# Which side of a runtime branch stands first: the same two blocks in the other order on three engines

## The chip, the cores and the metric

The kernel runs on one core of a Trainium2 chip. Its measure is the device time of one launch in microseconds (us). Each engine of the core (TensorE, VectorE, ScalarE, GpSimd, SyncE) has its own instruction stream and runs it in order; between engines only semaphores order the work. Instructions are fetched from memory while the program runs, and the profile shows these fetches as DMA queues of their own kind, "instruction".

## The reference

Three stages in float32: attention, a soft mixture of 8 experts, and a gated layer.

```python
scores = scale * q @ k.T                         # 2 x 8 heads, 768 positions, 64 wide
keep = (pos_k < n_sink) | ((rel >= 0) & (rel < window))
a = softmax(where(keep, scores, -1e9));  x = a @ v
P = exp(x @ w_gate - max);  8 times: rows, then columns normalised
out = sum over e of P[:, e] * (relu(x @ w1[e]) @ w2[e])
return ((out @ w_a) * (out @ w_b)) @ w_out
```

`n_sink` and `window` are inputs, here 4 and 128. With at most 16 sinks and a window of 1 to 129 the non-zero part of the scores is a narrow band and 16 columns; with other values it can be anything.

## The kernel before, in words

Since the two sizes are known only on the device, the kernel holds two forms of the attention stage. VectorE reads the sizes, computes `in_range` (1 when the band form is valid), and raises `range_ready`. Each engine then calls `chosen`, which waits for it and loads the value into a register. Two tests follow on each engine: `If(fits == 0)` with the general block (one head at a time over all 768 keys, in loops) and then `If(fits == 1)` with the sink-and-band block. For the inputs timed here the first test fails and the second holds. An engine therefore jumps over its general block, and runs through the sink-and-band block behind it into the rest.

The sink-and-band block handles 8 pairs of heads. Queries and keys are split into a high and a low part (ScalarE L956 and L958 make the high one, VectorE L1258 and L1261 the low one), TensorE multiplies three parts per tile of 128 queries (L541), VectorE adds the mask and takes the row minimum (L1272), ScalarE applies the exponential (L967), GpSimd and VectorE normalise, TensorE transposes (L567) and multiplies with the values (L588, L595). Ahead of the first pair VectorE also makes the mask: L1234 and L1236, then L1242 and L1245. Pairs overlap: while pair p is transposed, the scores of p + 2 are made.

Behind the branch TensorE makes the router's logits (L648), which VectorE copies out (L1373); then come the experts, in groups of 14 products (L623 to L625) on weight parts that VectorE and ScalarE split (L1336, L948) and whose results VectorE adds (L1535). Experts 1 to 6 run in a hardware loop of six turns (L1652 on VectorE, L824 on TensorE). SyncE issues the loads; those of the next weights wait for the splits of the last (`w_lo`). One wait inside the last step of the block matters below: L1331 is held until L1325 has ended (`t_sum`).

On VectorE the general block takes 280 rows of the program order (rows of equal neighbours are merged), on TensorE 117, on ScalarE 25, on SyncE 24, on GpSimd 8.

Of the kernel before, what the change touches and what calls it, by code (L numbers as in the profile page):

```python
# [33 lines left out]
def build(nc, qT, kT, v, sizes, w_gate, w1, w2, w_a, w_b, w_out, out):  # L34
    B, H, D, S = qT.shape
# [5 lines left out]
    KC = DM // P  # L41
# [14 lines left out]
    LEAD = 2  # L56
    RING = 4
    PAIRS = HEADS // 2
# [19 lines left out]
    with ctx:  # L78
        def sem(name):
            return ctx.enter_context(nc.semaphore(name))  # L80
# [92 lines left out]
        s = {n: sem(n) for n in names}  # L173
# [114 lines left out]
        @block.sync  # L288
        def _(sp):
            def load_pair(i, b):  # L290

                row = batch_rows(i, b)
                if i > 0:
                    sp.wait_ge(s["qk_lo"], 2 * (B * i + b - 1))
                sp.dma_start(rk[:, b].rearrange("d (t n) -> d t n", n=PITCH)[:, :, 0:P],
                             kT_rows[bass.ds(row, P), :].rearrange("d (t n) -> d t n", n=P))\
                    .then_inc(s[f"qk_in{b}"], 16)
                sp.dma_start(rq[:, b, :], qT_rows[bass.ds(row, P), :]).then_inc(s[f"qk_in{b}"], 16)

            def load_values(b):  # L300

                sp.dma_start(vs[:, b], v_rows[b][:, :, 0:P]).then_inc(s[f"v_in{b}"], 16)
                sp.wait_ge(s["sink_zero"], 1)
                sp.dma_start(vz[0:SINK, b], v_rows[b][0:SINK, 0, 0:P]).then_inc(s[f"v_in{b}"], 16)

            def load_w1(e, hf, sub):
                f0 = hf * FM * P + sub * SUBF
                sp.dma_start(raw1[:, sub], w1_rows[:, bass.ds(e * KC, KC), f0:f0 + SUBF])\
                    .then_inc(s[f"raw1_in{sub}"], 16)

            def load_w2(e, hf):
                sp.dma_start(raw2[:], w2_rows[:, bass.ds(e * HALVES * FM + hf * FM, FM), :])\
                    .then_inc(s["raw2_in"], 16)

            def load_step(e, hf):
                n = HALVES * e + hf
                for sub in range(2):
                    sp.wait_ge(s["w_lo"], 6 * (n - 1) + 3 * sub + 3)
                    if not isinstance(e, int):
                        sp.sem_inc(s["past"])  # L320
                    load_w1(e, hf, sub)
                sp.wait_ge(s["w2_lo"], FM * n)
                if not isinstance(e, int):
                    sp.sem_inc(s["past"])
                load_w2(e, hf)

            def general_loads(j, c, b):
                group = (j * KC + c) * B + b
                row = batch_rows(c, b)
                sp.wait_ge(s["d_lo"], 2 * group + 2)  # L330
                sp.sem_inc(s["past"])
                sp.dma_start(d_q, qT_rows[bass.ds(row, P), bass.ds(j * P, P)]).then_inc(s["d_in"], 16)
                sp.dma_start(d_k, kT_rows[bass.ds(row, P), :]).then_inc(s["d_in"], 16)
                sp.dma_start(d_v, v_rows[b][:, :, bass.ds(c * P, P)]).then_inc(s["d_in"], 16)


            sp.dma_start(ints[:], sizes.bitcast(I32).rearrange("(a n) -> a n", a=1).to_broadcast([P, 4]))\
                .then_inc(s["flags_in"], 16)
            load_pair(0, 0)
            load_pair(0, 1)  # L340
            load_values(0)
            sp.dma_start(wg[:], w_gate.rearrange("(c p) e -> p c e", p=P)).then_inc(s["gate_in"], 16)
            fits = chosen(sp)
            with sp.If(fits == 0):
                for landed in ("qk_in0", "qk_in1"):
                    sp.wait_ge(s[landed], 32)
                sp.wait_ge(s["v_in0"], 32)
                for sub in range(2):
                    load_w1(0, 0, sub)
                with sp.Fori(0, QT) as j:  # L350
                    with sp.Fori(0, KC) as c:
                        for b in range(B):
                            general_loads(j, c, b)
                sp.wait_ge(s["d_lo"], 2 * GROUPS + 2)
                load_w2(0, 0)

            with sp.If(fits == 1):
                load_values(1)
                for sub in range(2):
                    load_w1(0, 0, sub)  # L360
                for i in range(1, KC):
                    for b in range(B):
                        load_pair(i, b)
                sp.wait_ge(s["qk_lo"], 2 * PAIRS)
                load_w2(0, 0)
            load_step(0, 1)
            with sp.Fori(1, E) as e:
                load_step(e, 0)
                load_step(e, 1)

            for t in range(STEPS2):
                for sub, rows in ((0, wa_rows), (1, wb_rows)):
                    sp.wait_ge(s["w_lo"], 6 * (STEPS + t - 1) + 3 * sub + 3)
                    sp.dma_start(raw1[:, sub], rows[:, :, t * SUBF:(t + 1) * SUBF])\
                        .then_inc(s[f"raw1_in{sub}"], 16)
                sp.wait_ge(s["w2_lo"], FM * STEPS + 2 * t)
                half = 2 * (t % 2)
                sp.dma_start(raw2[:, half:half + 2], wo_rows[:, 2 * t:2 * t + 2, :]).then_inc(s["raw2_in"], 16)


            for x in range(TILES):
                t = x if x < HTILES else HTILES + ORDER[x - HTILES]
                sp.wait_ge(s["out_acc"], HTILES * (KT - B) + x + 1)
                sp.dma_start(out_rows[:, t, :], acc[:, t, :]).then_inc(s["out_sent"], 16)
            sp.wait_ge(s["out_sent"], 16 * TILES)
# [537 lines left out]
        def _(act):  # L923
# [7 lines left out]
            def gate_parts_hi():  # L931
                act.wait_ge(s["gate_in"], 16)
                nc.scalar.copy(wgs[:, :, 0:E], wg[:]).then_inc(s["gate_hi"], 1)
                nc.scalar.copy(wgs[:, :, GL:GL + E], wg[:]).then_inc(s["gate_hi"], 1)
# [15 lines left out]
            def split_pair_hi(p):  # L950
                i, b = divmod(p, B)
                q_hi, _, k_hi, _ = pair_parts(b)
                if p >= 2:
                    act.wait_ge(s["scores"], 2 * QT * (p - 1))
                act.wait_ge(s[f"qk_in{b}"], 32 * (i + 1))
                nc.scalar.copy(q_hi, rq[:, b, :]).then_inc(s["qk_hi"], 1)  # L956
                act.wait_ge(s["sinks_in"], p + 1)
                nc.scalar.copy(k_hi, rk[:, b, 0:KW]).then_inc(s["qk_hi"], 1)  # L958
# [66 lines left out]
                                     accum_out=esum[:, 0, 0:1]).then_inc(s["d_exped"], 1)  # L1025

            fits = chosen(act)
            with act.If(fits == 0):
                with act.Fori(0, QT) as j:
                    with act.Fori(0, KC) as c:  # L1030
                        for b in range(B):
                            for a in range(2):
                                general_head(j, c, b, a)
                act.wait_ge(s["d_t"], 1)
                nc.scalar.copy(xoh_op[:, 4, :], x32_op[:, 5, :]).then_inc(s["d_thi"], 1)
                act.wait_ge(s["d_t"], 5)
                nc.scalar.copy(xoh_op[:, 0:2, :], x32_op[:, 0:2, :])
                nc.scalar.copy(xoh_op[:, 3, :], x32_op[:, 3, :])
                nc.scalar.copy(xoh_op[:, 2, 0:BEFORE_LAST], x32_op[:, 2, 0:BEFORE_LAST])
                nc.scalar.copy(xoh_op[:, 5:7, 0:BEFORE_LAST], x32_op[:, 5:7, 0:BEFORE_LAST])\  # L1040
                    .then_inc(s["d_thi"], 1)
                act.sem_inc(s["t_hi"], 10)
                gate_parts_hi()
                ws_hi(0, 0, (0, 1, 2))

            with act.If(fits == 1):
                for p in range(LEAD):
                    split_pair_hi(p)
                for p in range(-LEAD, PAIRS):
                    if p == -1:  # L1050
                        gate_parts_hi()
                    pair(p)

            def gate_exp():

# [143 lines left out]
        def _(dve):  # L1199
# [223 lines left out]
                nc.vector.tensor_copy(x32_flat[rows, bass.ds(at, P)], ps[rows, O_BANK, 0:P]).then_inc(s["d_lo"], 1)  # L1423

            fits = chosen(dve)
            with dve.If(fits == 0):
                dve.wait_ge(s["d_pos"], 2)
                for jh in range(2):
                    with dve.Fori(0, QT // 2) as j3:
# [30 lines left out]
                dve.sem_inc(s["x_ready"], 1)  # L1460
                gate_parts_lo()
                ws_lo(0, 0, (0, 1, 2))

            with dve.If(fits == 1):
                in_window()
                split_pair_lo(0)
                make_mask()
                mask_scores(0, (0, 1))
                split_pair_lo(1)
                for p in range(-LEAD, PAIRS):  # L1470
                    if p == -1:
                        gate_parts_lo()
                    pair(p)


            links = 0
# [323 lines left out]
```

## Time and profile before

| | us |
|---|---|
| median of 3 runs | 1452.02 (1451.71 to 1453.65) |
| the profiled execution | 1450.18 |
| its span, first to last instruction | 1448.4 |
| TensorE busy | 1398.6 (97%) |
| VectorE busy | 808.4 (56%) |
| ScalarE busy | 501.5 (35%) |
| GpSimd busy | 223.7 (15%) |

Instruction queues in the whole span: q8 with 36 packets of 0.59 MB together, q14 with 24 of 0.20 MB. A load of half a step's weights is 512.0 KB and lands 3.4 us after its issue (median of 32).

A profile records one execution. The busy shares say which engine is full over the whole span; which engine sets the time of a short stretch is read from the chain of waits in that stretch. An idle time put down to "issue" is one for which the profile shows no semaphore that came late.

### The profile page before, as it was taken

The page shows a single profiled execution, that of the slowest core. Times are in us where ns is not written, and L with a number is a line of the kernel's source. Part 1 is how long each engine was busy: PE and PEld are TensorE (multiplying, and loading weights), DVE is VectorE, ACT ScalarE, POOL GpSimd, SP SyncE. Part 2 cuts the span into 40 slices and gives each one's busy share as a digit, 9 for nine tenths or more (in the row PEclk, how much of TensorE's full clock was granted, in tenths as well). Part 3 has the DMA queues.
Part 4 walks back from the last instruction along what each step waited for, and adds up shares of the span by engine and source line. Part 5 has one row for each costly group of instructions (what it writes and reads, how often), then busy time and mean ns, then how long its engine had stood idle before and what let it go on. Part 6 is the DMA issues. An engine that isn't in the chain of part 4 may idle for free.

```text
span 1448.4 us, 20715 instructions
## 1 busy us (share of the span) xinstructions
PE 1398.6 (97%) x7400; PEld 1246.1 (86%) x7400; DVE 808.4 (56%) x1585; ACT 501.5 (35%) x1085; POOL 223.7 (15%) x289
## 2 busy tenths in 40 slices
PE   4877999999999999999999999999999999999999
PEld 3655889988889998889998888998888989999998
DVE  6898765645444453544545444454544666656665
ACT  5785232423223242222323222242322443232331
POOL 3355110101101010110101011010111321101100
PEclk9999999999999999999999999999999999999999
DMA  4311100001010000101001010000100001001002
GB/s 141 100 45 56 44 30 29 30 29 59 15 44 29 29 29 29 58 21 37 29 29 32 26 58 29 29 29 29 58 15 29 15 30 44 30 30 44 30 1 88
DMA packets 49724, 56.45 MB, mean 39 GB/s; under 512 B 2432, under 2 KB 37376, under 8 KB 49664
## 3 DMA queue, kind: packets, MB, share of 16 engines
q1 hardware_dynamic: 44768, 53.26, 11.3%
q10 hardware_dynamic: 4896, 2.41, 0.6%
q8 instruction: 36, 0.59, 0.2%
q14 instruction: 24, 0.20, 0.0%
HBM read 52.51 MB, written 3.15 MB: 38 GB/s over the span
## 4 chain that ended last, share of the span: by engine, by line
PE 86%; DVE 7%; ACT 4%; issue 2%; DMA 0%; DVEq 0%; ACTq 0%
PE ps L623 28%; PE ps L625 28%; PE ps L624 28%; ACT pr L967 2%; DVE pr L1298 1%; DVE st L1675 1%; DVE pr L1272 1%; DVE wsl L1336 1%; PE ps L693 1%; DVE pt L1307 1%; ACT pt L976 1%; PE ps L567 0%; ACT st L1139 0%; ACT hh L1146 0%; DVE acc L1714 0%
## 5 line engine op out<-in xcount | busy, mean ns | idle before, releaser
L623 PE MATMUL ps<-xoh,wsh 128*128 128x384 f32 x1232 | 414.9, 337 | 3.0 <-DVE xol L1579 2.1
L625 PE MATMUL ps<-xol,wsh 128*128 128x384 f32 x1232 | 412.7, 335 | 0.0
L624 PE MATMUL ps<-xoh,wsl 128*128 128x384 f32 x1232 | 412.3, 335 | 0.0
L623 PE MATMUL ps<-w2h,hh 128*128 128x512 f32 x912 | 360.7, 396 | 0.8 <-DVE acc L1557 0.8
L625 PE MATMUL ps<-w2l,hh 128*128 128x512 f32 x912 | 359.8, 395 | 0.0
L624 PE MATMUL ps<-w2h,hl 128*128 128x512 f32 x912 | 359.6, 394 | 0.0
L1562 DVE SCALAR_TENSOR_TENSOR acc<-ps,g_now,acc 128x512 f32<-128x512 f32 x180 | 135.1, 751 | 201.7 <-PE ps L625 201.7
L623 PEld LDWEIGHTS ps<-xoh,wsh 128*128 128x128 f32 x1232 | 231.3, 188 | 10.5 <-DVE st L1675 3.9
L624 PEld LDWEIGHTS ps<-xoh,wsl 128*128 128x128 f32 x1232 | 231.3, 188 | 3.7
L625 PEld LDWEIGHTS ps<-xol,wsh 128*128 128x128 f32 x1232 | 231.2, 188 | 0.0
L625 PEld LDWEIGHTS ps<-w2l,hh 128*128 128x128 f32 x912 | 171.7, 188 | 39.8
L623 PEld LDWEIGHTS ps<-w2h,hh 128*128 128x128 f32 x912 | 171.9, 188 | 37.0 <-DVE acc L1557 1.2
L624 PEld LDWEIGHTS ps<-w2h,hl 128*128 128x128 f32 x912 | 171.8, 188 | 35.7
L436 POOL TENSOR_TENSOR sst<-raw 128x256 f32<-128x256 f32 x44 | 32.5, 738 | 1037.6 <-DVE wsl L1336 1037.6
L1071 ACT COPY st<-ps 128x384 f32<-128x384 f32 x96 | 46.0, 480 | 373.7 <-PE ps L625 373.7
L1535 DVE TENSOR_TENSOR st<-ps,st 128x384 f32<-128x384 f32 x96 | 53.4, 557 | 122.2 <-PE ps L625 122.2
L1535 DVE TENSOR_TENSOR ab<-ps,ab 128x384 f32<-128x384 f32 x96 | 53.5, 558 | 85.0 <-PE ps L625 84.9
L1543 DVE SCALAR_TENSOR_TENSOR hl<-ps,hh 128x384 fp32r<-128x384 f32 x64 | 35.7, 557 | 77.2 <-ACT hh L1084 76.7
L1336 DVE TENSOR_TENSOR wsl<-raw,wsh 128x512 fp32r<-128x512 f32 x88 | 63.8, 739 | 17.4 <-ACT wsh L948 17.4
L948 ACT CAST wsh<-raw 128x512 fp32r<-128x512 f32 x88 | 52.0, 621 | 55.2 <-POOL raw L438 55.2
L1084 ACT ACTIVATE hh<-ps 128x384 fp32r<-128x384 f32 x64 | 31.5, 491 | 106.1 <-PE ps L625 106.1
L1071 ACT COPY ab<-ps 128x384 f32<-128x384 f32 x96 | 46.1, 480 | 55.6 <-PE ps L625 55.6
(142 smaller groups left out, 1337.8 us busy)
## 6 DMA issues: line engine op xcount, KB each, us to landing
raw<-in_w_dram SPq DMA_DIRECT2D x32, 512.0 KB, 3.4
raw<-in_w_dram SPq DMA_DIRECT2D x16, 1024.0 KB, 5.1
rk<-in_k_dram SPq DMA_DIRECT2D x8, 384.0 KB, 4.0
rq<-in_q_dram SPq DMA_DIRECT2D x8, 384.0 KB, 4.9
raw<-in_w_a_dram SPq DMA_DIRECT2D x6, 512.0 KB, 3.6
raw<-in_w_b_dram SPq DMA_DIRECT2D x6, 512.0 KB, 3.6
raw<-in_w_out_dram SPq DMA_DIRECT2D x6, 512.0 KB, 3.5
out_dram<-acc SPq DMA_DIRECT2D x12, 256.0 KB, 2.0
```

What stands on the lines that cost most here:

```text
L436: nc.gpsimd.tensor_tensor(s1, a21, a22, ALU.add).then_inc(s["s_sum"], 1)
L623: nc.tensor.matmul(o, ah, bh, start=first, stop=False, skip_group_check=True)
L624: nc.tensor.matmul(o, al, bh, start=False, stop=False, skip_group_check=True)
L625: return nc.tensor.matmul(o, ah, bl, start=False, stop=last, skip_group_check=True)
L948: nc.scalar.copy(ws_piece(wsh, sub, j), ws_raw(sub, j)).then_inc(s["w_hi"], 1)
L967: nc.scalar.activation(t, t, ACT.Exp, bias=nmin[:, r, j:j + 1], scale=-1.0, accum_out=esum[:, r, j:j + 1]).then_inc(s["exped"], 1)
L1071: nc.scalar.copy((st, ab)[sub][:, slot, :], ps[:, bank_of(sub, name), 0:HT]).then_inc(s["kept"], 1)
L1084: nc.scalar.activation(hh[:, 2 * sub + 1, 0, :], ps[:, bank_of(sub, "P4"), 0:HT], ACT.Relu)\
L1336: nc.vector.tensor_tensor(ws_piece(wsl, sub, j), ws_raw(sub, j), ws_piece(wsh, sub, j).bitcast(F32), ALU.subtract)\
L1535: nc.vector.tensor_tensor(t, ps[:, bank_of(sub, name), 0:HT], t, ALU.add).then_inc(s["c_add"], 1)
L1543: nc.vector.scalar_tensor_tensor(out=hl[:, 2 * sub + m, half, :], in0=src, scalar=0.0, in1=hh[:, 2 * sub + m, half, :].bitcast(F32), op0=A ...
L1562: ins = nc.vector.scalar_tensor_tensor(out=acc[:, tile, :], in0=ps[:, Y_BANK + k % 2, :], scalar=g_now[:, tile:tile + 1], in1=acc[:, tile, ...
```

## The change

On VectorE, ScalarE and SyncE the two `If`s become one `If(fits == 1)` with an `Else`: the sink-and-band block stands first and the general block behind it. Nothing inside the blocks changes. TensorE and GpSimd keep the two `If`s with the general block first. In the diff the moved blocks are cut.

```diff
@@ SyncE
-            with sp.If(fits == 0):
+            with sp.If(fits == 1):
+                load_values(1)
...
+                load_w2(0, 0)
+            with sp.Else():
                 for landed in ("qk_in0", "qk_in1"):
...
-            with sp.If(fits == 1):
-                load_values(1)
...
@@ ScalarE
-            with act.If(fits == 0):
+            with act.If(fits == 1):
+                for p in range(LEAD):
+                    split_pair_hi(p)
+                for p in range(-LEAD, PAIRS):
+                    if p == -1:
+                        gate_parts_hi()
+                    pair(p)
+            with act.Else():
                 with act.Fori(0, QT) as j:
...
@@ VectorE
-            with dve.If(fits == 0):
+            with dve.If(fits == 1):
+                in_window()
+                split_pair_lo(0)
+                make_mask()
+                mask_scores(0, (0, 1))
+                split_pair_lo(1)
+                for p in range(-LEAD, PAIRS):
+                    if p == -1:
+                        gate_parts_lo()
+                    pair(p)
+            with dve.Else():
                 dve.wait_ge(s["d_pos"], 2)
...
-            with dve.If(fits == 1):
-                in_window()
...
```

The line numbers behind the blocks fall by 2 or 3 (VectorE's L1234 becomes L1232, its L1373 becomes L1371).

The order on VectorE at its first test, before: the test L1426 stands in front of the general block, and the second test L1464 in front of the band block.

```order
L202 ISA x2
L1426 COMPARE_AND_BRANCH
L1429 UNCONDITIONAL_BRANCH
L1429 ISA
...
L1336 TENSOR_TENSOR wsl<-sst,wsh 128x768
L1426 UNCONDITIONAL_BRANCH
L1464 COMPARE_AND_BRANCH
L1234 TENSOR_SCALAR pt<-pt,lim 128x672
L1236 SCALAR_TENSOR_TENSOR pt<-pt 128x672
```

The same place after the change.

```order
L202 ISA x2
L1424 COMPARE_AND_BRANCH
L1232 TENSOR_SCALAR pt<-pt,lim 128x672
L1234 SCALAR_TENSOR_TENSOR pt<-pt 128x672
L1256 TENSOR_TENSOR wsl<-rq,wsh 128x768
```

The 280 rows between the first test and the mask's first step are gone from there, and one test with them.

The order on VectorE at the end of the band block, before: the last outputs of the attention (L1331), then the copies of the logits (L1373); the unconditional branch goes to the row behind it.

```order
L1329 TENSOR_TENSOR x<-ps,x 128x384
L1331 TENSOR_TENSOR x<-ps,x 128x384
L1464 UNCONDITIONAL_BRANCH
L1373 COPY lt<-ps 40x384 x2
L1336 TENSOR_TENSOR wsl<-raw,wsh 128x512 x2
```

After: the same branch now has 279 rows between it and its target.

```order
L1327 TENSOR_TENSOR x<-ps,x 128x384
L1329 TENSOR_TENSOR x<-ps,x 128x384
L1424 UNCONDITIONAL_BRANCH
L1437 UNCONDITIONAL_BRANCH
...
L1334 TENSOR_TENSOR wsl<-sst,wsh 128x768
L1434 UNCONDITIONAL_BRANCH
L1371 COPY lt<-ps 40x384 x2
L1334 TENSOR_TENSOR wsl<-raw,wsh 128x512 x2
```

The general block has moved here from in front of the band block. On TensorE both orders are the same but for the line numbers.

## Rows read from the trace of the kernel before

**Rows 1.** The page, part 4: the chain that ended last, by engine.

```profile
PE 86%; DVE 7%; ACT 4%; issue 2%; DMA 0%; DVEq 0%; ACTq 0%
```

**Rows 2.** The waits from 0 to 24 us: who waited, total, times, longest.

```profile
PE ps L541 <- DVE wsl L1261: 14.6, 1, 14.6
DVE pt L1234 <- issue: 6.4, 1, 6.4
```

**Rows 3.** The chain from 0 to 24 us: start, duration, what.

```profile
5.90 5.29 issue
11.29 0.58 DVE pt L1234
...
13.62 0.95 DVE wsl L1261
...
15.98 0.29 DVE pr L1272
```

**Rows 4.** Branches by line: duration in ns min/median/max, first and last start in us.

```profile
L1426 DVEq COMPARE_BRANCH  x1: 67/67/67, 5.8 to 5.8; - x1
...
L1464 DVEq COMPARE_BRANCH  x1: 50/50/50, 11.2 to 11.2; - x1
...
L697 PEldq COMPARE_BRANCH  x1: 5560/5560/5560, 5.9 to 5.9; - x1
...
L1046 ACTq COMPARE_BRANCH  x1: 40/40/40, 5.8 to 5.8; - x1
```

**Rows 5.** Instruction queues from 9.0 to 9.5 us: packets, MB, share of 16 engines.

```profile
q8 instruction: 1, 0.02, 11.7%
q14 instruction: 1, 0.01, 3.9%
```

**Rows 6.** Windows: busy of PE, PEld, DVE, ACT, POOL, clock, DMA share, GB/s.

```profile
5.80:11.20 5.40, 0.00 (x0) 0.00 (x0) 0.00 (x0) 3.26 (x4) 0.50 (x2) 1.00 0.98 290
```

**Rows 7.** The timeline from 7 to 17 us: start, duration, engine, line, what.

```profile
7.43 0.89 ACT L958 CAST wsh<-rk 128x848 fp32r<-128x848 f32 x1
...
14.63 0.47 PE L541 MATMUL ps<-wsh,wsl 64*128 64x128 f32 x2 [14.63 <-DVE wsl L1261]
...
15.12 0.41 PE L541 MATMUL ps<-wsh 64*128 64x128 f32 x2
...
15.89 0.43 PE L541 MATMUL ps<-wsh 64*128 64x272 f32 x2
...
16.41 0.44 DVE L1272 CUSTOM_DVE_ANT_0 pr<-ps,mask 128x272 f32<-128x272 f32 x1
```

**Rows 8.** VectorE's backward branch of the expert loop.

```profile
L1652 DVEq COMPARE_BRANCH  x6: 50/56/74, 403.1 to 1029.4; - x6
```

**Rows 9.** Instruction queues from 403.7 to 404.3 us.

```profile
q14 instruction: 1, 0.01, 4.4%
```

**Rows 10.** The timeline of VectorE from 403 to 408 us.

```profile
405.80 0.56 DVE L1535 TENSOR_TENSOR st<-ps,st 128x384 f32<-128x384 f32 x1 [1.97 <-PE ps L625]
```

**Rows 11.** Windows, columns as in rows 6.

```profile
139.90:141.10 1.20, 1.20 (x8) 1.20 (x8) 1.20 (x4) 0.00 (x0) 1.20 (x2) 1.00 0.88 252
```

**Rows 12.** The wait instruction in front of L1325, on VectorE's sequencer.

```profile
L1324 DVEq EVENT_SEMAPHORE  x4: 21/21/21, 97.8 to 136.8; - x4
```

**Rows 13.** The timeline from 138.7 to 149.4 us, VectorE and GpSimd.

```profile
139.21 0.54 DVE L1325 TENSOR_TENSOR x<-ps,x 128x384 f32<-128x384 f32 x1
...
141.07 0.54 DVE L1373 COPY lt<-ps 40x384 f32<-40x384 f32 x1
...
142.98 2.94 DVE L1336 TENSOR_TENSOR wsl<-raw,wsh 128x512 fp32r<-128x512 f32 x2 [0.59 <-ACT wsh L948]
...
143.90 1.47 POOL L456 TENSOR_TENSOR xol<-x,xoh 128x384 fp32r<-128x384 f32 x1
...
145.84 0.95 DVE L1336 TENSOR_TENSOR wsl<-sst,wsh 128x768 fp32r<-128x768 f32 x1
```

**Rows 14.** The waits from 138 to 160 us.

```profile
PEld ps L623 <- DVE st L1535: 0.4, 1, 0.4
```

More of the change, by code:

```diff
@@ L343, in _ @@
             fits = chosen(sp)
-            with sp.If(fits == 0):
+            with sp.If(fits == 1):
+                load_values(1)
+                for sub in range(2):
+                    load_w1(0, 0, sub)
+                for i in range(1, KC):
+                    for b in range(B):
+                        load_pair(i, b)
+                sp.wait_ge(s["qk_lo"], 2 * PAIRS)
+                load_w2(0, 0)
+            with sp.Else():
                 for landed in ("qk_in0", "qk_in1"):
@@ L354, in _ @@
                 sp.wait_ge(s["d_lo"], 2 * GROUPS + 2)
-                load_w2(0, 0)
-            with sp.If(fits == 1):
-                load_values(1)
[L359 to L364, printed above, removed]
                 load_w2(0, 0)
@@ L1044, in _ @@
                 ws_hi(0, 0, (0, 1, 2))
[L1046 to L1052, printed above, removed]
             def gate_exp():
@@ L1462, in _ @@
                 ws_lo(0, 0, (0, 1, 2))
-            with dve.If(fits == 1):
-                in_window()
[L1466 to L1473, printed above, removed]
             links = 0
```

## The prediction, written before the changed kernel ran

> **What bounds the kernel now.** I read the page first. The chain that ended last is 86% TensorE, so a change on the other engines can only pay where TensorE stands idle [rows 1]. The list of waits for the first 24 us shows that place. TensorE does not start its first matmul until 14.6 us, because it waits for the last of VectorE's key splits (L1261), and VectorE itself sat idle 6.4 us before L1234, with no releaser that the profile shows ("issue") [rows 2]. The chain of the same stretch then runs on VectorE alone: 5.29 us of issue from 5.90, L1234 at 11.29, L1261 at 13.62, the first masked scores at 15.98 [rows 3]. Those 5.29 us are what the change is about.
>
> The branch instructions say what they are [rows 4]. VectorE's first test (L1426) is executed at 5.8 and costs 0.067; its second (L1464) is executed only at 11.2. Between them it jumps over the general block, which is 280 rows of its program. TensorE's first test (L697), which jumps 117 rows, is itself recorded as 5.560 us, from 5.9 to 11.45. ScalarE and GpSimd jump 25 and 8 rows, and ScalarE's second test is already at 5.8. So a short jump costs about 0.1 us and a long one about 5.4. The instruction queues carry one packet each just then, q8 and q14, inside a window of 0.5 us from 9.0 [rows 5]: the code at the target was not there and had to be fetched, 3.4 us after the jump, over DMA engines that were 98% busy [rows 6]; some 1.6 us after the packet the engine went on.
>
> **The change part by part.** *VectorE's first jump goes.* It now falls into L1234 right behind its test. What else it needs: nothing released L1234 [rows 2], so the positions it reads were there, and ScalarE's splits end when L958 begins, at 7.43, and at 7.43 + 0.89 = 8.32 [rows 7]. So L1234 starts at about 5.95 (5.8, the test's 0.067, and the little that lay between test and instruction at 11.2), the first split on VectorE follows ScalarE's at about 7.5, and L1261 starts at about 8.4 and takes 0.95: 9.4 [rows 3]. From its end (14.57) to the first masked scores (15.98) lay 1.41 of mask steps, which makes 10.8. VectorE would be 5.1 us early.
>
> *TensorE's jump stays.* It comes out at 11.45, and its next instructions (a second test, a semaphore) take it to about 11.85. Until now that was hidden below the wait to 14.63; now it is the later of the two (11.85 against 9.4) and sets the start. TensorE gains 14.63 - 11.85 = 2.8. VectorE's first masked scores need the third pair of matmuls of tile 0, which starts 0.49 after the first (15.12 against 14.63) and takes 0.41: 11.85 + 0.90 = 12.75. The second tile's pair starts 1.26 after the first (15.89) and runs 0.43 [rows 7]: 13.58. Before, the masking of that tile started at 16.41 [rows 7], so 2.8 is left there. From there on the chain is exps, splits and normalisation on engines that all start from these events; the key and query loads wait for VectorE's splits and move along with them. I carry 2.8 to the end of the attention stage. Bounds: 5.1, if TensorE's fetch became free too (then VectorE's own work is the limit); 0, if a later wait took it all.
>
> *VectorE gets a jump at the end of its block*, over the general block that now lies there, 279 rows of the order, to L1371 (L1373 before). No row shows a jump at that place, so it is bounded. From above: 5.35, the first jump, under full DMA. From below: behind the loop's first backward branch at 403.1 [rows 8] a packet went inside a window from 403.7 [rows 9], some 0.7 after the branch, between loads; 0.7 + 0.3 + the 1.6 of above is 2.6. Here the load of the next weights is on its way: DMA share 0.88 from 139.9 to 141.1 [rows 11]. I take 3.3, nearer to the idle end because that is one load of 512 KB, and such loads land after a median of 3.4, where the first jump met one load behind another.
>
> What hides it: VectorE's sequencer runs ahead. The semaphore instruction in front of L1325 was executed at 136.8 [rows 12] and L1325 started at 139.21 [rows 13]. The last instruction that can hold the jump back is L1331, which waits for L1325 (done at 139.21 + 0.54 = 139.75). So the jump starts at about 139.9 on the old clock and VectorE is back at 143.2 (142.5 to 145.2). Queued behind it: two copies of logits (from 141.07), three splits of the second half of the weights (from 142.98), then the first additions. The two splits at 142.98 took 2.94 together, where the third, half as wide again, took 0.95, so 0.63 would be theirs; GpSimd was at work beside them until 145.37 [rows 13]. Copies from 143.2 end at 144.15; the first split then runs against GpSimd until about 145.4, and the other two take 0.6 and 0.9, so the third ends near 147.0, against 145.84 + 0.95 = 146.8 before. Who waits: TensorE needs the splits for its seventh product; its eighth already waits 0.4 for VectorE's additions [rows 14], and gets the whole delay. I take 0.3; the ends are 0 (back at 142.5) and 1.4 (back at 145.2: copies to 146.1, splits of 0.6, 0.6 and 0.9 to 148.2).
>
> *ScalarE and SyncE* swap 25 and 24 rows. Their early jumps cost about 0.1 [rows 4]. Their new jumps at the end are as short as the ones whose price is known. I take 0, bounds -0.1 and +0.1. GpSimd and TensorE keep their order.
>
> **The sum**, against the profiled execution: span 1448.4 - 2.8 + 0.3 = 1445.9, and 1450.18 around it becomes 1447.7. The median of the runs shown is 1452.02, 1.8 above the profiled one; less 2.5 it is 1449.5.
>
> *A rule weighed against this.* The Trainium skill (Runtime: NRT & Kernel Launch, "Instruction fetch mechanics") says that a taken branch whose target is outside the fetched window stalls on a DMA, that blocks are 16 KiB and that the window is 512 instructions, 2048 on TensorE. By that rule TensorE's jump over its general block would have been inside its window; its 5.560 us say otherwise [rows 4]. By the same window VectorE's end jump could be inside too and cost nothing, and the sum would be -2.8 instead of -2.5. I follow the first jump, which was not free.
>
> **The rivals.**
> 1. *TensorE's start moves further.* For: its fetch and VectorE's went at the same time, and only one is left. Against: 3.4 us of waiting lay behind data packets, which stay. Then VectorE's mask is the limit and up to 5.1 is won; halfway, 4 less 0.3: 1448.3.
> 2. *The end jump costs as much as the first.* For: a burst of loads is under way. Against: it is 512 KB and not several loads. Then -2.8 + 1.4 = -1.4: 1450.6.
> 3. *Nothing is won.* Either the 5.3 us are no jump, or the attention stage absorbs the earlier start, for instance in its loads. Against: the two tests at 5.8 and 11.2. 1452.0.
> 4. *Slower: the loop loses its place.* VectorE's loop of 246 rows turns back six times at about 0.06 us [rows 8], so it is held complete. It now stands one instruction earlier, since the second test is gone. If it fell over one block more than is held, each turn would fetch: the branch is at 403.1 and the next instruction that matters is at 405.80 [rows 10], so it decides from a stall of 2.7. At 5.35 it would add 2.65 six times, 15.9, less 2.5: about 1465. Against: a shift by one instruction seldom crosses a border.
>
> **How the numbers follow.** Forecast 0.60, with a range of its own from 1448.6 to 1450.2; rival 1 0.12, rival 2 0.16, rival 3 0.06, rival 4 0.06. No change that a measurement can tell is within 0.2%, 2.9 us, so 1449.1 is the border; the forecast lies close to it. Of its 0.60 I give 0.25 to the faster side; with rival 1 that is 0.37. Same: 0.35 + 0.16 + 0.06 = 0.57. Slower: 0.06. The range leaves out rival 4 and the far end of rival 1: 1447.8 to 1451.6.
>
> **What would show it.** Right: VectorE's L1232 (was L1234) near 6, TensorE's first matmul near 11.9 while its first test still takes about 5.5; the first masked scores near 12.8; the logits kept back by VectorE, two copies about 2 us late on the shifted clock, with a packet on q14 ahead of them; the eighth product's wait 0.3 longer; the loop still (1029.4 - 403.1) / 5 = 125.3 us a turn [rows 8]. Wrong: a first matmul at 14.6 or below 10 (the jump of TensorE is not what sets the start), VectorE's copies in place (no end stall) or more than 4 us late, or packets on q14 in the loop.

## The result, and the profile after

| | before | after |
|---|---|---|
| median of 20 runs each, us | 1451.68 (1449.38 to 1453.65) | 1449.01 (1447.14 to 1450.59) |
| ratio | | 0.9983 [0.9977, 0.999] |
| profiled execution, us | 1450.18 | 1447.26 |
| its span, us | 1448.4 | 1445.4 |

The change gains 2.7 us, 0.17%; forecast were 2.5. I read the start first. The chain by engine is still TensorE's [rows 1]:

```profile
PE 88%; DVE 6%; ACT 4%; issue 2%; DMA 0%; SPq 0%; POOL 0%; DVEq 0%; ACTq 0%
```

The waits from 0 to 24 us of the changed kernel (who waited, total, times, longest), which answer to [rows 2]:

```profile
PE ps L540 <- issue: 11.7, 1, 11.7
...
DVE pt L1232 <- issue: 1.0, 1, 1.0
```

VectorE's 6.4 us before its first mask step are down to 1.0, and the first matmul is no longer held by VectorE's split but by "issue", at 11.7 instead of 14.6. The chain of the same stretch (start, duration, what), against [rows 3]:

```profile
8.46 1.05 DVE wsl L1259
9.52 2.22 issue
11.73 1.71 PE ps L540 x12
13.44 0.43 DVE pr L1270
```

The split that the matmul needs ends at 9.52; for 2.22 us more TensorE alone keeps the chain. The branches by line (duration in ns min/median/max, first and last start) say with what, as in [rows 4]:

```profile
L696 PEldq COMPARE_BRANCH  x1: 5483/5483/5483, 5.9 to 5.9; - x1
```

```profile
L1424 DVEq COMPARE_BRANCH  x2: 50/56/63, 5.8 to 136.7; - x2
```

TensorE's jump still takes 5.48. VectorE's test falls through at 5.8 in 0.05, and its second execution, at 136.7, is the new jump at the end of the block. The timeline of the start, VectorE:

```profile
5.93 0.57 DVE L1232 TENSOR_SCALAR pt<-pt,lim 128x672 f32<-128x672 f32 x1 [1.04 <-issue]
...
8.46 1.04 DVE L1259 TENSOR_TENSOR wsl<-rk,wsh 128x848 fp32r<-128x848 f32 x1
...
10.37 0.51 DVE L1243 TENSOR_SCALAR mask<-pt 128x672 f32<-128x672 f32 x1
12.78 0.29 DVE L1270 CUSTOM_DVE_ANT_0 pr<-ps,mask 128x128 f32<-128x128 f32 x1 [1.89 <-PE ps L540]
```

The mask is ready at 10.9 and VectorE waits 1.89 us for TensorE. Now the end of the block, VectorE and GpSimd from 136 to 147 us, against [rows 13]:

```profile
136.12 0.56 DVE L1323 TENSOR_TENSOR x<-ps,x 128x384 f32<-128x384 f32 x1
...
137.52 0.55 DVE L1329 TENSOR_TENSOR x<-ps,x 128x384 f32<-128x384 f32 x1
...
140.36 1.01 DVE L1371 COPY lt<-ps 40x384 f32<-40x384 f32 x2 [2.29 <-issue]
141.30 1.27 DVE L1334 TENSOR_TENSOR wsl<-raw,wsh 128x512 fp32r<-128x512 f32 x2
142.50 0.95 DVE L1334 TENSOR_TENSOR wsl<-sst,wsh 128x768 fp32r<-128x768 f32 x1
...
145.53 0.56 DVE L1532 TENSOR_TENSOR st<-ps,st 128x384 f32<-128x384 f32 x1 [0.48 <-PE ps L624]
```

```profile
140.84 4.55 POOL L455 TENSOR_TENSOR xol<-x,xoh 128x384 fp32r<-128x384 f32 x1
```

The instruction queue from 138.3 to 138.9 us (packets, MB, share):

```profile
q14 instruction: 1, 0.01, 4.2%
```

The branch is executed at 136.7, ahead of the last addition (L1329, 137.52), because the sequencer runs ahead of the engine, but not before L1323, the addition that L1329 waits for, has ended (136.12 + 0.56 = 136.68). The packet follows 1.8 us later, and the copies start at 140.36, 3.6 us behind the branch. On the shifted clock their place was 141.07 - 2.83 = 138.2. They are 2.1 late, and yet the splits behind them are done at 143.45, where 146.8 - 2.83 = 144.0 would have been their old place: the first two take 1.27 together, not 2.94, and it is GpSimd's operation that takes 4.55, not 1.47. Before, VectorE had also stood idle for 0.23 in front of its second copy and for 0.59 in front of the splits; late as it is now, it finds both ready. The third of the following additions even waits 0.48 for TensorE. TensorE's eighth product, before and after (timeline of TensorE):

```profile
149.20 0.44 PE L623 MATMUL ps<-xoh,wsh 128*128 128x384 f32 x1
```

```profile
146.37 0.33 PE L622 MATMUL ps<-xoh,wsh 128*128 128x384 f32 x1
```

It starts 2.83 earlier, and its wait for VectorE [rows 14] has no row any more (that this is not the change's doing is shown under "What the end jump costs" below). From here the lead stays: the loop's branch goes from 403.1 to

```profile
L1649 DVEq COMPARE_BRANCH  x6: 50/56/75, 400.1 to 1026.4; - x6
```

and a turn takes (1026.4 - 400.1) / 5 = 125.3 us, as before [rows 8].

One thing blurs single profiles. The granted clock of TensorE falls to its lower level for 3.4 us twice in either kernel's attention stage, but not in the same place: before at 58.3 and 106.0 us, after at 102.9 and 130.2. The same ten microseconds at the end of attention, before and then after (window, busy of PE, PEld, DVE, ACT, POOL, clock, DMA share, GB/s):

```profile
128.00:138.00 10.00, 7.16 (x59) 4.78 (x58) 7.29 (x11) 5.28 (x10) 3.69 (x3) 1.00 0.01 2
```

```profile
128.00:138.00 10.00, 8.16 (x56) 6.25 (x55) 7.91 (x12) 3.94 (x7) 5.40 (x5) 0.83 0.13 36
```

A clock of 0.83 over ten microseconds is 3.4 at half. Number, length and place of such falls differ from profile to profile below, so the verdicts rest on medians.

### The profile page after: what moved, and what is told of

It is laid out like the page before. It is cut to its first block, busy times and chain, and to the rows that moved or that the text cites. A ratio compares the mean times of both kernels' runs of the same rounds, so it can differ in the third digit from the quotient of the medians.

```text
span 1445.4 us, 20715 instructions
## 1 busy us (share of the span) xinstructions
PE 1399.2 (97%) x7400; PEld 1247.1 (86%) x7400; DVE 807.8 (56%) x1585; ACT 502.0 (35%) x1085; POOL 228.6 (16%) x289
## 4 chain that ended last, share of the span: by engine, by line
PE 88%; DVE 6%; ACT 4%; issue 2%; DMA 0%; SPq 0%; POOL 0%; DVEq 0%; ACTq 0%
PE ps L622 29%; PE ps L624 28%; PE ps L623 28%; ACT pr L966 2%; DVE pr L1296 1%; DVE st L1672 1%; DVE pr L1270 1%; PE ps L692 1%; ACT pt L975 1%; PE ps L647 0%; DVE pt L1305 0%; PE ps L566 0%; ACT st L1137 0%; ACT hh L1144 0%; DMA rq<-in_q_dram 0%
```

## The experiments

Every ratio is against the kernel before, timed on the same chip between the runs. A kernel is called "after" or "before" plus its one edit.

**1. VectorE alone.** Before, with only VectorE's two blocks exchanged.

```diff
-            with dve.If(fits == 0):
+            with dve.If(fits == 1):
...
-            with dve.If(fits == 1):
+            with dve.Else():
```

> Only VectorE has the sink-and-band block first; ScalarE and SyncE are as before. Theory (VectorE's long jump is what held the start): all of the gain is there, ratio to before 0.998 (-2.7 us, -2 to -3.5), first matmul at 11.7 us, as after the whole change. Rival (part of it comes from ScalarE's or SyncE's side, whose second test and early loads move by 0.1 to 0.2 us): less than two thirds of it, -1.8 us or less.

Measured: 1448.88 against 1451.18, ratio 0.9982 [0.9973, 0.9991]. The timelines of TensorE, VectorE and GpSimd in this kernel:

```profile
11.63 0.47 PE L541 MATMUL ps<-wsh,wsl 64*128 64x128 f32 x2 [11.63 <-issue]
```

```profile
142.66 1.01 DVE L1373 COPY lt<-ps 40x384 f32<-40x384 f32 x2 [2.47 <-issue]
143.59 1.28 DVE L1336 TENSOR_TENSOR wsl<-raw,wsh 128x512 fp32r<-128x512 f32 x2
```

```profile
142.94 4.03 POOL L456 TENSOR_TENSOR xol<-x,xoh 128x384 fp32r<-128x384 f32 x1
```

VectorE's edit holds the whole of the change, both its sides and the exchange between VectorE and GpSimd at the end.

**2. ScalarE and SyncE alone.** The same edit on `act` and `sp`, VectorE as before.

```diff
-            with act.If(fits == 0):
+            with act.If(fits == 1):
...
-            with sp.If(fits == 0):
+            with sp.If(fits == 1):
```

> Only ScalarE and SyncE have the sink-and-band block first; VectorE is as before. Theory (their general blocks are short, so neither jump costs anything): no difference, ratio 1.000 within its interval, first matmul at 14.6 us. Rival (a taken jump over an Else costs ScalarE at the end of its block, in front of the last token parts): ratio 1.001 or more.

Measured: 1451.44 against 1450.81, ratio 1.0004 [0.9995, 1.0013]: no difference that can be measured, as in the sum.

**3 and 4. How far is far?** One run each: before, with VectorE's jump made shorter by rolling up one level of the general block's loops; then the same with 32 instructions more in that block. They are not executed here.

```diff
-                for jh in range(2):
+                with dve.Fori(0, 2) as jh:
...
+                for _ in range(32):              # only in the second
+                    dve.sem_inc(s["past"])
```

> Order of before; VectorE's general block half rolled, so that its first jump goes from instruction 21 of its program to 190 (before: 330; with rolled loops: 131, which cost 0.6 us). Nothing is left out. Theory (what counts is whether the block of 128 instructions, 8 KB, that holds the target is loaded; two are at the start, the packets of 8 KB say): second test executed by 6.5 us, L1234 near 6.6, no packet for VectorE before it. Rival (the stall grows with the distance): second test at 8 us or later.

> The kernel with the half rolled block, and 32 semaphore increments more at the end of VectorE's general block, which is not executed: the target moves from instruction 190 to 222. Theory (the border of the two loaded blocks lies between them, since packets came when VectorE crossed instruction 450 and 578 of its old program, which puts a border at 194): the full stall of 3.5 to 5.4 us, second test at 9.5 to 11.2 us, with a packet on q14 in front. Rival (32 instructions more change nothing): second test by 6.6 us.

Measured: 1448.18 and 1449.79; with one run each, the traces are the evidence and not the times. VectorE's first and second test with the nearer target, then the second test with the farther one, whose first is at 5.6 too:

```profile
L1426 DVEq COMPARE_BRANCH  x1: 67/67/67, 5.6 to 5.6; - x1
...
L1464 DVEq COMPARE_BRANCH  x1: 50/50/50, 6.2 to 6.2; - x1
```

```profile
L1466 DVEq COMPARE_BRANCH  x1: 50/50/50, 11.0 to 11.0; - x1
```

The first matmul of either, in the same order:

```profile
11.58 0.47 PE L541 MATMUL ps<-wsh,wsl 64*128 64x128 f32 x2 [11.58 <-issue]
```

```profile
14.43 0.47 PE L541 MATMUL ps<-wsh,wsl 64*128 64x128 f32 x2 [14.43 <-DVE wsl L1261]
```

With its target at VectorE's instruction 190 the jump costs 0.6 us; with it at 222, 5.4. The kernel before has 5.4 for a target at 330, and experiment 5 has 0.6 for one at 131. That is no price per instruction, it is a step, as if the code at the target were there or not. A packet goes on q14 at 9.1 in both kernels; only the one with the farther target stands still until after it. The nearer target also gives the changed kernel's start with the order of before, so what the change wins is this stall and nothing about the order as such.

**5. Both fetches taken away, order of before.** The general blocks of TensorE and VectorE in fully rolled loops, with the same work for other sizes: 74 and 108 instructions to jump over.

```diff
-                for jh in range(2):
-                    with pe.Fori(0, QT // 2) as j3:
-                        for kh in range(2):
-                            with pe.Fori(0, 2) as kk:
+                with pe.Fori(0, QT) as j:
+                    with pe.Fori(0, KC) as c:
...
-                for jh in range(2):
+                with dve.Fori(0, 2) as jh:
...
-                        for kh in range(2):
+                        with dve.Fori(0, 2) as kh:
```

> Order of before (general block first everywhere), but the general blocks of TensorE and VectorE are written with rolled loops, so that TensorE jumps over 74 instructions of its program instead of 284 and VectorE over 108 instead of 308. Nothing is left out. Theory (a jump is dear only when its target is far enough not to be loaded yet): both jumps cost 0.1 us, no packet on the instruction queues between 6 and 11 us, the first matmul at about 9.5, the first masked scores at about 10.9, no jump at the end: -5.1 us, ratio 0.9965. Rival (a taken branch over a block stalls whatever its length while loads fill the DMA engines): first matmul still at 11.7 to 14.6, ratio 0.998 to 1.0.

Measured: 1446.32 against 1451.18, ratio 0.9965 [0.9951, 0.9978]: 4.9 us by the medians, 5.1 by the ratio. TensorE's first branch, the timeline of its start, and that of VectorE and GpSimd at the end:

```profile
L697 PEldq COMPARE_BRANCH  x1: 372/372/372, 5.9 to 5.9; - x1
```

```profile
9.86 0.47 PE L541 MATMUL ps<-wsh,wsl 64*128 64x128 f32 x2 [9.86 <-DVE wsl L1259]
```

```profile
138.20 0.55 DVE L1371 COPY lt<-ps 40x384 f32<-40x384 f32 x1 [0.75 <-PE ps L648]
138.83 2.94 DVE L1334 TENSOR_TENSOR wsl<-raw,wsh 128x512 fp32r<-128x512 f32 x2
```

```profile
137.94 1.85 POOL L453 TENSOR_TENSOR xol<-x,xoh 128x768 fp32r<-128x768 f32 x1 [0.24 <-ACT xoh L997]
139.75 1.47 POOL L456 TENSOR_TENSOR xol<-x,xoh 128x384 fp32r<-128x384 f32 x1
```

With TensorE's own jump at 0.37 the first matmul waits for VectorE again, at 9.86: the rest of the start was TensorE's fetch. VectorE's first jump costs 0.6 here (5.8 to 6.4), not the 0.1 that I expected. I had also expected no packets between 6 and 11 us, and there I was wrong: one goes on q14 at 8.9 and one on q8 at 9.3, while VectorE and TensorE go on without a stop. So a packet near a jump does not show by itself that the engine waited for it. With the copies in time, the splits take their old 2.94 and GpSimd its 1.47.

**6. After, with TensorE's block rolled.** The first half of the edit of 5, on the changed kernel; VectorE keeps its far jump at the end.

> The changed kernel, and TensorE's general block (still first) with rolled loops: 74 instructions to jump over. VectorE keeps its long jump at the end of its block. Theory (after the change TensorE's jump alone sets the start, and VectorE's end jump is hidden): first matmul at about 9.5, masked scores at about 10.9, -1.9 us against the changed kernel and -4.6 to -5.1 against before; VectorE's copies of the logits still come 2 us late. Rival (VectorE's end jump takes part of what the start wins): -3.5 us or less against before, clearly behind the kernel with both blocks rolled.

Measured: 1446.32, ratio 0.9963 [0.9951, 0.9975]. The first matmul is at 9.63. VectorE and GpSimd at the end:

```profile
140.14 1.01 DVE L1369 COPY lt<-ps 40x384 f32<-40x384 f32 x2 [2.10 <-PE ps L647]
141.08 1.28 DVE L1332 TENSOR_TENSOR wsl<-raw,wsh 128x512 fp32r<-128x512 f32 x2
```

```profile
140.80 3.30 POOL L455 TENSOR_TENSOR xol<-x,xoh 128x384 fp32r<-128x384 f32 x1
```

The list names TensorE as what released the copies, but the branch is at 136.69 and the copies 3.45 behind it, as in the changed kernel: a wait for several things is put down to one of them. The far jump at the end is there, the splits are short, GpSimd's operation is long again, and the time is that of 5. So it costs nothing that these times can tell (their intervals reach about 2 us to either side).

**7. After, with both blocks rolled.** The whole edit of 5 on the changed kernel.

> The changed kernel with the general blocks of TensorE and VectorE in rolled loops (74 and 109 instructions). Nothing is left out. Theory: VectorE has no jump at the start and a short one at its end, TensorE a short one at the start: first matmul at about 9.3 to 9.6 us, copies of the logits in place, and since VectorE's end jump was hidden anyway, no more than 0.5 us better than the rolled kernels run so far: ratio to before 0.9963, between 0.995 and 0.997. Rival (the long end jump of VectorE did cost something): 1.5 us or more better than those, ratio 0.9955 or less.

Measured: 1446.9 against 1450.81, ratio 0.9964 [0.995, 0.9978]. Copies in place (138.13), splits 2.94, and no better than 5 or 6. With an interval of 2 us to either side this rules out that VectorE's end jump costs several microseconds; that it costs next to nothing is read from the traces (below). Nor does the order of the blocks show any worth once the jumps are short.

**8. All five engines band first.** After, with TensorE and GpSimd exchanged too.

```diff
             fits = chosen(pe)
-            with pe.If(fits == 0):
-                for jh in range(2):
...
             with pe.If(fits == 1):
...
+            with pe.Else():
+                for jh in range(2):
```

> All five engines have the sink-and-band block first. Theory (TensorE's own jump at the start, 5.5 us, is the limit left; a jump over the general block costs 3 to 5 us wherever it stands, and counts where the engine has no slack): the first matmul moves from 11.7 to about 9.5 and the first masked scores from 12.8 to about 10.9, another 1.9 us won; but TensorE now jumps at the end of its block, in front of the logits, where it has 0.6 us or less of idle time: 2 to 3.5 us lost. Ratio to before 0.998 to 1.0 (-2.7 to 0 us), that is, no better than the change itself. Rival (TensorE's queue of matmuls hides its end jump as VectorE's was hidden): -4.5 us, ratio 0.997.

Measured: 1452.88 against 1451.18, ratio 1.0011 [1.0002, 1.002], slower than before, and by more than I expected. TensorE's timeline has the start as promised, its branches are these, and the end looks like this:

```profile
9.26 0.47 PE L539 MATMUL ps<-wsh,wsl 64*128 64x128 f32 x2 [9.26 <-DVE wsl L1257]
```

```profile
L695 PEldq COMPARE_BRANCH  x2: 98/2218/4338, 5.9 to 130.4; - x2
```

```profile
131.69 0.84 PE L593 MATMUL ps<-pt,vz 128*64 128x384 f32 x4
134.92 0.41 PE L646 MATMUL ps<-xoh,wgs 128*128 128x384 f32 x1 [2.39 <-issue]
139.28 0.48 PE L646 MATMUL ps<-xol,wgs 128*128 128x384 f32 x1 [3.95 <-issue]
139.55 0.52 PE L646 MATMUL ps<-xoh,wgs 128*128 128x384 f32 x1
```

and the windows of that stretch:

```profile
137.10:144.00 6.90, 4.72 (x15) 4.72 (x15) 0.55 (x1) 2.22 (x5) 2.77 (x3) 0.51 0.01 4
144.00:150.00 6.00, 6.00 (x36) 6.00 (x36) 4.36 (x6) 2.90 (x6) 2.25 (x3) 1.00 0.20 64
```

The start gains 14.63 - 9.26 = 5.4. At the end the branch takes 4.34 us, from 130.4 on. Matmuls that were already queued cover part of it: TensorE works until 131.69 + 0.84 = 132.53 and then stands idle for 2.39, where in the kernel before it idles for 0.66 too (it waits for GpSimd). So the branch costs 1.7 of its 4.34. One matmul runs; then TensorE stops again for 3.95. The program has no wait between these two matmuls, nothing releases the second, and TensorE's instruction queue (q8) carries another packet at 136.98. That second stop I had not expected, and nothing covers it. TensorE's granted clock is at its lower level (1.2 GHz) from 137.1 to 144.0, and matmuls of 0.33 take 0.52. That the stop brought the clock down is not shown: falls of the same 6.8 us stand in the attention stage of experiments 1, 6 and 7 too, with no such stop.

**9. The same order with rolled blocks.** Experiment 8 with the edit of 5.

> All engines have the sink-and-band block first and the general blocks of TensorE and VectorE are rolled (74 and 109 instructions to jump over at the end of the block). Nothing is left out. Theory (what made the kernel with all blocks first slower was TensorE's end jump to code that was not loaded, and the slow clock behind its idle time; a near target costs 0.1 to 0.6 us): no jump left at the start, first matmul at about 9.3 us, TensorE's end branch under 0.6 us instead of 4.3: ratio to before 0.996 (0.9945 to 0.9975), as good as the best so far. Rival (a jump at the end of TensorE's block stalls in front of the logits whatever its length): 2 us or more behind those, ratio 0.998 or more.

Measured: 1445.76 against 1450.55, ratio 0.9964 [0.9951, 0.9978]. TensorE's branch at the end is at 130.19 and takes 0.18. The loss of 8 was the distance of the jumps, not the order. GpSimd's exchange, which 8 and 9 have beside TensorE's, is not the cause either.

**10. A second far jump of VectorE at the end.** After, with a test that fails behind the join and 300 instructions to jump over, none of which is executed.

```diff
+            with dve.If(fits == 0):
+                for _ in range(300):
+                    dve.sem_inc(s["past"])
             links = 0
```

> The changed kernel, with a second test and a jump over 300 instructions that are never executed, on VectorE right behind the join: the suspected cost at the end doubled. Theory (the first jump's stall was hidden by VectorE's sequencer running ahead and by slack of about 0.5 us in front of TensorE's eighth product): the copies of the logits come another 2.6 to 3.6 us late, the splits end 2.7 us later, and TensorE waits for VectorE: 1.7 to 3 us lost against the changed kernel, ratio to before 0.9995 to 1.0005. Rival (VectorE has several us of room there): ratio 0.998, as the changed kernel.

Measured: 1452.71 against 1450.55, ratio 1.0014 [1.0005, 1.0023]. Against the changed kernel that is 3.7 us by the medians and 4.5 by the two ratios, more than I expected. VectorE's timeline, and the waits from 135 to 160 us:

```profile
146.26 1.01 DVE L1371 COPY lt<-ps 40x384 f32<-40x384 f32 x2 [5.95 <-issue]
147.20 1.27 DVE L1334 TENSOR_TENSOR wsl<-raw,wsh 128x512 fp32r<-128x512 f32 x2
```

```profile
PE ps L622 <- DVE wsl L1334: 2.1, 1, 2.1
...
PE ps L622 <- DVE st L1535: 1.0, 1, 1.0
```

The tests are executed at 138.97 and 142.82 and the copies at 146.26: a second stall of 3.4. TensorE loses 3.1 of them in two waits. The splits take 1.27 here because GpSimd had finished, at 143.06 + 1.01 = 144.1. So the first far jump was hidden, but used up nearly all of the cover. What lies between 3.1 and the measured 3.7 to 4.5 isn't shown; TensorE's own first jump took 6.20 us in this profile (5.48 in that of after), which is 0.7, and by experiment 2's profile (6.12) it varies on its own.

## Why the prediction was right

- **What bounds the start.** Right. VectorE's first mask step moved from 11.29 to 5.93 (forecast 5.95). VectorE was ready at 10.9 (10.8), and was not the limit. TensorE's own jump was: first matmul at 11.73 (11.85), first masked scores at 12.78 (12.75). Experiments 1, 3 and 4 show that a stall of VectorE's fetch had held the start, 5 and 6 that TensorE's holds the rest. Taking one fetch away did not help the other: TensorE's jump took 5.56, 5.80 and 6.12 beside a far jump of VectorE (before, experiments 4 and 2) and 5.38, 5.48, 5.52 and 6.20 without one (experiment 1, after, experiments 3 and 10). So rival 1 falls.
- **The lead is carried.** Right. 2.9 at the first matmul, 3.0 at the masking of the second tile (16.41 to 13.43, forecast 2.8), 2.83 at the eighth product, 3.0 at the loop. Between them it was smaller for a while: the logits' first matmul starts at 138.06 before and 135.50 after, 2.56. The clock fell in another place in the two profiles (after, from 130.2, just ahead of the logits); whether that is the reason I have not shown. Rival 3 falls.
- **The end jump's stall.** Right: 3.6 from the branch where I took 3.3 (2.6 to 5.35), with its packet, and copies 2.1 late for a forecast of 2. The wait that I named holds the branch: it comes 0.05 us behind the end of L1323, and just as close behind the same addition in experiments 1, 6, 7 and 10. In time it was 136.7 and not 139.9 - 2.8 = 137.1, because this addition is earlier by 3.1 and not by 2.8, and I had added 0.15. Start and stall are off by 0.4 and 0.3 in opposite directions, so that the copies come where I had them is partly luck. The lower bound of 2.6 had no ground: it took the packet near 403.8 for the fetch of the loop's backward branch, but VectorE's next instruction (L1642) had already started at 403.67, and in experiment 3 the same branch turns back at 400.8 with no packet of q14 near it (the nearest are at 378.7 and 1033.6).
- **What the end jump costs.** The size of this term was wrong: 0.3 forecast, 0 measured. My step was "the first split then runs against GpSimd until about 145.4, and the other two take 0.6 and 0.9", with the third split ending near 147.0 on the old clock. It ends at 143.45 + 2.83 = 146.3. Of the 2.1 that VectorE comes late, 1.0 is made up in front of the splits, most of it where VectorE had idled before, so the splits start 1.15 late (141.30 + 2.83 = 144.13 against 142.98). Then the runs show an exchange: where VectorE comes late, its splits run at full speed from the first on (1.27 for two) and GpSimd's operation is the one that stretches, to 3.3 to 4.6; where VectorE is in time, two splits take 2.94 and GpSimd 1.47. Late, with 1.27 or 1.28: after, 1 and 6. In time, with 2.93 or 2.94: before, 2, 3, 4, 5, 7 and 9. The exchange gives 1.7 back, more than the 1.15, and the splits are done half a microsecond ahead of their old place.

  From the first matmul of the logits to the eighth product TensorE takes 10.87 us after the change (135.50 to 146.37), 10.86 in experiment 5 and 10.87 in 7, which have no far jump, and 11.14 before. So the jump costs nothing in this profile, and what it is shorter than 11.14 is not its doing either. The profiles without the 0.4 of wait [rows 14] are those in which the clock was low shortly before the logits; in the ones where it was not (before, 2, 4 and 9) the wait is there, and none of these has VectorE's one far jump at the end. What that jump would cost there is not shown. Rival 2 falls here, though experiment 10 shows that it was near: 3.4 more of delay cost 3.1.
- **ScalarE and SyncE.** Right (experiment 2).
- **The loop.** Right: 125.3 us a turn. Rival 4 falls.
- **The sum.** 1449.5 forecast and 1449.0 measured; -2.5 forecast, -2.7 by the medians, -2.9 in the profiled executions (1450.18 to 1447.26). The 0.3 of the end jump is within what is left over. I gave the greater chance (0.57) to a change within 0.2%; at 0.17% it is that, by little.

The price of a jump is what the row of the branch, or the gap to the next row, says; a packet by itself says nothing (experiment 5). The Trainium skill (Runtime: NRT & Kernel Launch, "Instruction fetch mechanics") gives its kind rightly, a step at the edge of what has been fetched, and experiments 3 and 4 agree (0.6 and 5.4 us for 32 instructions of difference). Its sizes don't fit: it says blocks of 16 KiB on every engine and 512 instructions held, 2048 on TensorE. Here q14 brought 0.20 MB in 24 packets, 8 KB each, against 16 KB for q8, and both a target at VectorE's instruction 222 and TensorE's first jump were outside. The end jump, which could have been free by that rule, stalled 3.6 us, and what made it cost nothing was its cover.

## What to carry to other kernels

A block that is never executed still costs: if a jump over it leads beyond the code that has been fetched, the engine stops for 3.4 to 6.2 us in these profiles, and an engine's branch row or the gap between its two tests shows it. Rolling the unexecuted block into loops, on the two engines where it is long, makes the jumps short (0.2 to 0.6 us) and beats every order of the long blocks that was run (-5 us here, against -2.7 for the change; nothing is left out). If the order is all that can be changed, put the jump where that engine has other engines' work to hide under, and count how much of that cover it uses: VectorE's end could hide one far jump and not two; TensorE's hid 2.6 of its branch's 4.3 us and nothing of the second stop behind it.

## What the runs showed of the hardware

- A far jump took 5.4 to 6.2 us at the start, beside DMA engines that are 98% busy [rows 6], and 3.4 to 4.3 at the end of attention. What differs is the time from the branch to its packet: 3.4 us at the start, 1.8 for VectorE's end jump, beside DMA engines 90% busy between 136.7 and 138.5, and 0.3 for TensorE's end jump of experiment 8, with the DMA engines 4% busy. VectorE goes on 1.8 to 1.9 us behind the packet, at the start and at the end. The shares go the same way as the times, but no run changed the load alone, so that the load is the cause is not shown.
- A short jump is not quite free: 0.6 us on VectorE (5.6 to 6.2 in experiment 3), 0.37 on TensorE at the start (experiment 5), 0.18 at the end (experiment 9).
- Behind a far jump a second stop can follow. TensorE had 4.34 us in the branch and 3.95 one matmul later, with a packet of its own (experiment 8).
- Of VectorE and GpSimd, run together on float32 operations with two inputs, one was slowed more than the other, and 2 us in VectorE's arrival decided which. Which began first does not settle it. In experiment 5 GpSimd was in L453 when VectorE's split began (137.94 and 138.83), and the split was the slow one. In experiment 6 GpSimd's L455 had begun before the split too (140.80 and 141.08), and this time GpSimd's operation was the slow one; VectorE had then been at work on its copies since 140.14. Undisturbed, two splits take 1.27 and GpSimd's operation 1.01 (experiment 10). Why the roles change stays open.
